# Local attention beside an MLP on one core: the mask added by the vector engine in PSUM, weight loads moved ahead of the first units' inputs, other orders at the end of the first units

## What is computed

```python
B, H, S, D, factor = 4, 8, 576, 64, 4
# pooled part: means over groups of 4 positions, full softmax attention over 144 positions, repeated 4 times
out_up = np.repeat(sm_attn(mean4(q), mean4(k), mean4(v)), factor, axis=2)
# local part: only keys nearer than 4 positions
mask = np.abs(pos[:, None] - pos[None, :]) < factor
scores = np.where(mask, scale * q @ k.T, -1e9)
out_local = softmax(scores) @ v
x = (out_up + out_local) as 2304 rows of 512
h = x @ w_in;   g = h - tanh(h);   y = g @ w_out        # w_in 512x2048, w_out 2048x512
h = y @ w2_in;  g = h * cos(h);    out = g @ w2_out
```

## Time and profile before

| what | value |
|---|---|
| device time, median of 3 runs | 917.86 us (917.54 to 923.1) |
| device time of the profiled execution | 918.26 us |
| span of the profiled execution | 916.1 us |
| TensorE busy | 903.7 us, 99% of the span |
| vector engine busy | 522.8 us, 57% |
| scalar engine busy | 376.0 us, 41% |
| pool engine busy | 146.4 us, 16% |
| bytes moved by DMA | 59.57 MB |

### The profile page before, as it was taken

The page is one execution under the profiler, slowest core; times in us unless marked ns, Lnnn a source line. Parts: engine busy times, 40 slices in busy tenths (PEclk is TensorE's granted clock), DMA queues, the critical chain, the costliest instruction groups (busy, mean ns, idle before and its releaser), DMA issues.

```text
span 916.1 us, 15863 instructions
## 1 busy us (share of the span) xinstructions
PE 903.7 (99%) x6264; PEld 838.9 (92%) x6264; DVE 522.8 (57%) x1071; ACT 376.0 (41%) x1055; POOL 146.4 (16%) x167
## 2 busy tenths in 40 slices
PE   8899999999999999999999999999999999999998
PEld 6689999999999999999999999999999999898997
DVE  5733544444445434433334787777777777777775
ACT  6744443443344334422232444443443434443433
POOL 5587400200000100000079820000000000000000
PEclk9999999999999999999999999999999999999999
DMA  9692012821004600301134501001001000000000
GB/s 297 234 297 65 1 58 75 184 71 47 1 34 132 164 1 1 105 1 35 60 114 138 161 1 35 35 1 35 35 1 35 35 1 1 35 1 1 36 1 34
DMA packets 24637, 59.57 MB, mean 65 GB/s; under 512 B 2292, under 2 KB 5492, under 8 KB 24564
## 3 DMA queue, kind: packets, MB, share of 16 engines
q1 hardware_dynamic: 22212, 50.01, 15.9%
q0 software_dynamic: 2352, 8.55, 5.2%
HBM read 49.12 MB, written 9.44 MB: 64 GB/s over the span
## 4 chain that ended last, share of the span: by engine, by line
PE 96%; DMA 2%; DVE 1%; ACT 1%; issue 0%; POOL 0%; POOLq 0%
PE ps L488 44%; PE ps L533 22%; PE ps L514 22%; PE ps L406 2%; DMA qk<-qkx_in 2%; PE ps L446 1%; PE ps L457 1%; PE ps L415 1%; PE ps L389 1%; PE ps L424 1%; PE ps L430 1%; PE ps L401 1%; ACT ps L595 0%; DVE x L789 0%; DVE ps L737 0%
## 5 line engine op out<-in xcount | busy, mean ns | idle before, releaser
L488 PE MATMUL ps<-xh,wi_hi 128*128 128x384 f32 x768 | 261.9, 341 | 2.2 <-DVE gl L830 2.2
L488 PE MATMUL ps<-xh,wi_lo 128*128 128x384 f32 x768 | 258.0, 336 | 0.0
L488 PE MATMUL ps<-xl,wi_hi 128*128 128x384 f32 x768 | 257.3, 335 | 0.0
L488 PEld LDWEIGHTS ps<-xh,wi_hi 128*128 128x128 f32 x768 | 144.2, 188 | 9.4 <-DVE gl L830 2.5
L488 PEld LDWEIGHTS ps<-xl,wi_hi 128*128 128x128 f32 x768 | 144.3, 188 | 4.0
L488 PEld LDWEIGHTS ps<-xh,wi_lo 128*128 128x128 f32 x768 | 144.1, 188 | 0.0
L635 ACT ACTIVATE gh<-rem 128x384 fp32r<-128x384 f32 x96 | 50.5, 526 | 213.6 <-PE ps L533 141.7
L822 DVE TENSOR_TENSOR ps<-ps,fn 128x384 f32<-128x384 f32 x96 | 54.2, 565 | 144.3 <-ACT fn L623 143.4
L514 PE MATMUL ps<-gh,wo_hi 128*128 128x384 f32 x384 | 132.3, 345 | 0.0
L514 PE MATMUL ps<-gl,wo_hi 128*128 128x384 f32 x384 | 128.5, 335 | 0.0
L514 PE MATMUL ps<-gh,wo_lo 128*128 128x384 f32 x384 | 128.4, 334 | 0.0
(11 more groups left out here) (86 smaller groups left out, 1110.3 us busy)
## 6 DMA issues: line engine op xcount, KB each, us to landing
qk<-qkx_in SPq DMA_DIRECT2D x20, 512.0 KB, 4.8
wi_raw<-w_in_in SPq DMA_DIRECT2D x32, 256.0 KB, 5.1
wo_raw<-w_out_in SPq DMA_DIRECT2D x8, 1024.0 KB, 6.0
qkd<-qkf_in POOLq DMA_DIRECT2D x9, 576.0 KB, 7.0
vb<-vx_in SPq DMA_DIRECT2D x20, 256.0 KB, 3.1
y_between<-stage SPq DMA_DIRECT2D x6, 768.0 KB, 3.5
x<-y_between SPq DMA_DIRECT2D x6, 768.0 KB, 5.3
out<-stage SPq DMA_DIRECT2D x18, 256.0 KB, 2.1
```

Source lines behind the costliest of these rows:

```text
L488: mm = MM(ps[:, h_bank(s), 0:NT], w, xx[:, kc, :], start=(n == 0), stop=(n == last))
```

## The change

1. For units from 9 on the two products with the mask are left out, each product of q and k starts its own sum, and DVE adds the mask to the scores in PSUM (one `tensor_tensor` over 128 x 512, mask repeated eight times) before it takes the maximum. There are 15 such local units. The maximum waits for that addition through a new semaphore, `masked`.
2. SP issues the loads of w_out group 1, of w_in groups 2 and 3, and of w_out groups 2 and 3 ahead of v of unit 9, of the first transfer of batch 1's pooled input, and of q/k of unit 10. The waits of each load stay as they were.
3. In the drain PE does the transposes of unit 8 ahead of the mixes of units 7 and 8, and the last three idle products go; ACT rounds the fourth piece of w_in group 0 (`hi_of_in(0, 3)`) after the drain's evacuations.
4. In the MLP's first step ACT and DVE do `g_hi` and `g_lo` of step 0 before the exponentials and the normalising of unit 9.

```diff
@@ scores
+                    by_dve = u >= FIRST
                     masks = mask_r[:, :].unsqueeze(1).broadcast_to([P, 4, KW])
-                    for k in range(2):
+                    for k in range(0 if by_dve else 2):
                         MM(ps[:, bank + k, 0:256]..., eye_r[:, :], masks, start=True, stop=False)
...
-                                    start=False, stop=(slot % 4 == 3))
+                                    start=by_dve, stop=(by_dve or slot % 4 == 3))
@@ top_score
                 ve.wait_ge(scored, after(u + 1))
+                if u >= FIRST and u in LOCALS:
+                    mask = mask_r[:, :].bitcast(F32).unsqueeze(1).unsqueeze(1).broadcast_to([P, 2, 4, KW])
+                    nc.vector.tensor_tensor(scores_of(u), scores_of(u), mask, ALU.add).then_inc(masked, 1)
+                    ve.wait_ge(masked, after(LOCALS.index(u) - NL + 1))
@@ sync
             load_qk(FIRST)
-            load_first_of_four(1)
             load_wo(0, 1, w_out)
-            load_v(FIRST)
             load_wi(0, 2, w_in)
-            load_qk(FIRST + 1)
+            load_wi(0, 3, w_in)
+
             sp.wait_ge(v_added, after(2))
             load_wo(0, 2, w_out)
-            load_v(FIRST + 1)
-            load_wi(0, 3, w_in)
 
             sp.wait_ge(qk_summed, after(4))
             sp.wait_ge(mixed, after(2))
             load_wo(0, 3, w_out)
+            load_v(FIRST)
+            load_first_of_four(1)
 
             next_store = 0
+            load_qk(FIRST + 1)
+            load_v(FIRST + 1)
@@ tensor, first units
-                if 0 <= k - 2:
+                if 0 <= k - 2 and k < FIRST:
                     mixes(k - 2)
                 if 0 <= k - 1:
                     transposes(k - 1)
-            keep_warm(FILL[FIRST + 1], banks(5))
+                if k == FIRST:
+                    mixes(k - 2)
             mixes(FIRST - 1)
@@ scalar
-                if 5 <= k < FIRST:
+                if 5 <= k < FIRST - 1:
                     hi_of_in(0, k - 5)
...
+            hi_of_in(0, 3)
             split_x(0, 2)
...
-                if s == -AHEAD:
-                    exponentials(FIRST)
                 attention(2 * s + 1)
                 g_hi(s + AHEAD)
+                if s == -AHEAD:
+                    exponentials(FIRST)
@@ vector
-                if s == -AHEAD:
-                    guard(FIRST)
-                    invert(FIRST)
-                    normalise(FIRST)
                 attention(2 * s + 1)
                 g_lo(s + AHEAD)
+                if s == -AHEAD:
+                    guard(FIRST)
+                    invert(FIRST)
+                    normalise(FIRST)
```

More of the change, by code:

```diff
@@ L178, in build @@
         scored, transposed, mixed = sem("scored"), sem("transposed"), sem("mixed")
-        topped, maxed, guard_done, inverted, normed, gathered = (
-            sem("topped"), sem("maxed"), sem("guard_done"), sem("inverted"), sem("normed"), sem("gathered"))
+        masked, topped, maxed, guard_done, inverted, normed, gathered = (
+            sem("masked"), sem("topped"), sem("maxed"), sem("guard_done"), sem("inverted"), sem("normed"), sem("gathered"))
         exped, evacuated = sem("exped"), sem("evacuated")
@@ L686, in _ @@
                 tanh_of_h(s + AHEAD)
+                attention(2 * s + 1)
+                g_hi(s + AHEAD)
                 if s == -AHEAD:
                     exponentials(FIRST)
-                attention(2 * s + 1)
-                g_hi(s + AHEAD)
                 if s == -2:
@@ L725, in _ @@
         def _(ve):
-            for s in (normed, topped, maxed, guard_done, inverted, gathered, xl_done, g_done, gl_done, ev_dve,
+            for s in (normed, masked, topped, maxed, guard_done, inverted, gathered, xl_done, g_done, gl_done, ev_dve,
                       u_done, n_done, r1_done, r_done):
@@ L903, in _ @@
                 g_of_h(s + AHEAD)
+                attention(2 * s + 1)
+                g_lo(s + AHEAD)
                 if s == -AHEAD:
@@ L907, in _ @@
                     normalise(FIRST)
-                attention(2 * s + 1)
-                g_lo(s + AHEAD)
                 for t, steps in XL_AT.items():
```

## The result

The changed kernel takes **915.3 us** (median of 12 runs, 913.28 to 916.42); the kernel before, in 12 runs, 922.44 us (917.54 to 926.77). The ratio is 0.9926, 95% interval 0.9907 to 0.9946. The forecast ratio, 911.4 to 917.86, was 0.9930, and lies in that interval; the forecast time of 911.4, with its range of 909.0 to 914.5, does not hold. Two things came out otherwise: the 917.86 that it started from is not the usual time of the kernel before, and of the 6.5 us of the sum the two profiled executions, both at full clock, show 5.0 (918.26 to 913.28). That the ratio fits is luck: the medians fell by 7.1 us, 5.0 of them by what the sum is about and 2.1 because the changed kernel runs less often and less long at half clock, which the sum leaves out. The profiles first; the clock comes with the experiments.

A forecast was written before the change was run, and what follows sets the result against it. TensorE, busy 99% of the span, was taken as the bound. 2.5 (to `hidden(4)`) - 1.3 (POOL) + 2.4 (unit 11) + 2.9 (masks) = 6.5 us, from 918.26 to 911.8, less 0.4: 911.4, range 909.0 to 914.5.

The forecast's parts named there:

- The start of the sum, with half clock put at nothing: Whole kernel: sum starts from the profiled 918.26 us, median put 0.4 below it, clock taken as full.
- POOL's stall: At `hidden(4)`: POOL waits for its pooled input until 46.4, so TensorE waits about 1.3 us (0.4 to 2.3) for w_in pieces.
- Rival 2: POOL's input lands after 47.4, or its later pieces come late too: 1.5 to 3 us more, 913.5; chance 0.12.
- To `hidden(4)`: Drain and MLP's first steps: the new orders bring `hidden(4)` from 55.95 to 53.5, a gain of 2.5 us.
- Unit 11: Scores of unit 11: the 2.2 us wait for q/k goes, with 0.24 for the masks: 2.4 us gained.
- The masks: Local units from 9 on: each dropped mask pair saves 0.24 us, 2.9 for 12 units; DVE's addition costs nothing.
- Rival 4: Local units: dropping the mask products gains nothing, 3.6 us less, 915.0; chance 0.05.
- The rule weighed: DMA queues share engines round-robin: POOL's addition must not begin before 48.5, or q/k of unit 10 gets half the engines.
- Rivals 1: At `hidden(4)`: pooled input lands by 45, POOL does not hold TensorE, the 1.3 us stay: 910.1; chance 0.22.
- 3: At unit 10: q/k late because POOL's additions share the DMA, a wait of 1.5 us: 912.5; chance 0.06.
- 5: At POOL's wait: weights delay its input, no gain if landing at 52.7, 921.5 us if at 56.4; chance 0.04.
- 6: Mixes of unit 9 don't wait for ACT and POOL doesn't hold TensorE: 908.5; chance 0.06.

The follow-up runs named there:

- ten: Kernel before with four more idle products in the drain, ahead of the transposes and the mixes of unit 7: 919.96 us, ratio 0.9983.
- eleven: Kernel before with four idle products in the drain and nine in each of its two waits of 2.2 us: 918.98 us, ratio 0.9965.
- thirteen: Changed kernel with three more idle products in the drain, ahead of the transposes of units 7 and 8: 915.76 us, ratio 0.9945.
- four: Changed kernel with POOL's pooled input loaded ahead of w_out groups 2 and 3, v of unit 9 and q/k of unit 10 ahead of group 3: 911.47 us.
- six: Kernel four with two of ACT's roundings of w_in group 1 moved behind the evacuation of unit 9: 911.95 us, ratio 0.9898.
- eight: Kernel four with DVE adding the mask twice in each of the 15 local units: 912.06 us, ratio 0.9907.
- fourteen: Changed kernel with `contract(2)` ahead of `hidden(4)` in TensorE's order: 911.89 us, ratio 0.9892.
- experiment three: Kernel before with only the new orders in the drain and the MLP's first step, masks and loads as before: 919.48 us, ratio 0.9973.
- experiment twelve: Kernel before with the change's order of loads alone and four idle products in the drain: 917.73 us, ratio 0.996.
- kernel two: Kernel before with only SP's new order of loads: 920.85 us, ratio 0.999.
- five: Kernel before with nine idle products ahead of each of its two waits of 2.2 us: 922.22 us, ratio 1.0005.
- seven: Kernel six with three more idle products in the drain, ahead of the transposes of units 7 and 8: 909.87 us, ratio 0.9876.

## Why the prediction was right in its parts and wrong in its number

The forecast of 911.4 is 3.9 us too low: 0.4 because it was put below the profiled execution, 1.5 because the profiled executions differ by 5.0 and not by 6.5, and 2.0 because the median of the changed kernel lies that much above its profiled execution. The last is the largest, and it is the clock's.

**The start of the sum, with half clock put at nothing,** is the step that failed. "The median of the runs lies 0.4 below the profiled one" was true of three runs. Over 92 runs the median is some 4 us above it, and only one in five is at 1.000. Of the 12 runs of the changed kernel four were at 1.000 and took 913.28, 913.45, 913.78 and 916.02 us; seven were at 0.997 or 0.998, at 915.03 to 916.42, and the median, 915.3, is one of theirs. Three of the four lie in the range; the fourth shows that a run at full clock can be late as well, and nothing here says why. The prediction named "a granted clock below 1 in the drain" as a cost that it had not counted "as the trace shows it full with gaps of 2.2 us". One profiled execution at full clock could not show that. Experiments ten, eleven and thirteen show it: half clock can stand behind the drain's pauses, behind the waits of 2.2 us, and in the change behind the three for POOL. The drain's is rarer in the change (its lowest clock in 12 runs is 0.997; kernels four, six, eight and fourteen had one run in six at 0.994), and experiment three points to the orders; in its place comes the one behind POOL's pieces.

**POOL's stall**, 1.3 us, was the right mechanism and 2.3 in size. The last piece was done at 57.7 and not at 56.3: the landing came 0.7 later, POOL came to the first piece 0.2 later behind that, and the four pieces took 5.9 us instead of 5.4, because the wait of 0.48 that the prediction took out of the row was there again. The 1 us that it put between the last byte and the landing stands in no row. TensorE wanted the pieces 0.5 later than put, so 0.9 of the 1.4 reached it, and 0.1 is the last restart. Rival 2 comes nearest, but not by its own condition: it had the landing behind 47.4, and it was at 46.9. That its 913.5 is close to the 913.28 of the profiled execution is partly luck, since only 1.0 of the 1.5 us missing there is POOL's.

**To `hidden(4)`** 1.9 us instead of 2.5. Of the difference 0.5 lies before the place of the change: the very first scores took 1.97 us instead of 1.19 in that execution, and the transposes of unit 7, up to which nothing differs on TensorE, start at 31.99 instead of 31.48. The granted clock of those rows is 1.00 in both, and no row says why. It belongs to the pair of traces and not to the change, so the term was right: without it the gains are 3.4 at `hidden(2)` (3.4 forecast) and 2.4 at `hidden(4)`. The wait of the mixes of unit 9 for ACT was 0.57 (0.9 forecast). Kernel six takes it away and gains nothing, but there v of unit 9 lands at 47.7; in the change it had landed at 44.8, so whether an earlier ACT would pay with the change's own order of loads is not tested.

**Unit 11**, 2.4: 2.64 measured, by 2.28 ahead after 0.36 behind. Rightly put down to the loads, as experiment twelve shows by itself. What the sum did not say is how it and the orders depend on each other: the orders alone bring 0.8 us up to unit 11 and nothing in the time; the loads 2.3, the masks 2.85, and all three with POOL's pieces in time 7.6 (918.24 to 910.62, lowest runs side by side). What is left for the orders, by subtraction, is some 2.4, nearly all of it only behind the loads.

**The masks**, 2.9: 2.7 at twelve units. The additions follow at 0.73 us (0.75 taken), and the slack was as computed. Rival 4 is out.

**What was costed at nothing** and wasn't: the third pooled input, 0.35 us at 310 us. POOL issues its last addition 3.8 us earlier than before (300.30 instead of 304.10), but it takes 10.2 us instead of 9.7, and TensorE comes 4.5 earlier, where before it left 1 us of room. This wait is 0.4 and 1.2 us in kernels ten and eleven, whose loads are as before, so it is not the change's alone.

**The rule weighed**, from the Trainium skill ("DMA: Bandwidth & Descriptors", "Queues, rings and completion order"), is not tested here. The first addition was issued at 47.12, earlier than the 48.5 that the prediction wanted, and q/k of unit 10 landed at 49.1; but TensorE took it at 50.72 and did not wait.

Rivals 1, 3, 5 and 6 did not come. That POOL need not hold TensorE is shown by kernel four, without any such wait, at 911.5 in the median; kernel fourteen, with 0.9 us of it left, took 911.9.

Still open: why the same program gets the half clock in one run and not in the next; what else sets runs at full clock up to 3 us apart (in the eight profiles at 1.000 the transposes of unit 7 start anywhere from 31.02 to 32.45 us, though TensorE's products up to there are nearly the same); and why kernel two at clocks of 0.999 and 1.000 took 917.81 and 918.36 where kernel twelve reached 916.26.

## What to carry to other kernels

A profile at full clock is one draw: before a time is forecast from it, ask how many runs are like it, and give the short pauses of TensorE a price even where the trace shows them free. When a wait is to be removed, look for what is next in time on each engine (here a transfer behind 5 MB of weights for POOL, then v of unit 9), and put ready work of TensorE ahead of a late operand before moving the operand. Count the waits in the list and not only their sum: here each cost about 0.27 us more than it lists (three waits, 1.5 listed and 2.3 lost), so many short waits are dearer than they look (fourteen more and a longer one, 4.1 listed and 7.1 lost).

## What the runs showed of the hardware

The drain's small products with pauses of 0.2 to 0.8 us between them were followed by some 10 us at half clock in the profiles of kernels two and five (and, by the mean clocks of 0.9945 or less, in 51 of 92 runs of the kernel before). Three or four idle products of 128x512 in those pauses took that away: all 42 runs of kernels seven, ten, eleven and twelve were at 0.996 or more, and the lowest times of kernels ten and eleven (918.54 and 918.28) are within half a microsecond of the kernel before's (918.06 and 918.81). Behind a wait of 2.2 us about 3.4 us at half clock (0.66 of five us) followed in kernel ten, and 3 us behind the three waits for POOL in thirteen.

After idle time the first product of 384 columns lasts 0.44 us instead of 0.33, and the next follows 0.28 us later instead of 0.175. It does the same without idle time behind the small products of scores and mixes (48.41 and 48.69 in the change). A listed wait of 2.22 us moved the next product by 2.56 in the kernel before (42.17 to 44.73), where 0.175 is usual, and with the late second product cost 2.49: again 0.27 more than listed.
